# Attention on f32 operands as loaded, with first-layer tiles of 256 and four times 512 tokens, in a fused attention and two-MLP kernel

## What is computed

```
# attention: q, k, v are (4, 8, 576, 64), window 64
scores = scale * q @ k.T ; mask = (rel >= 0) & (rel < 64), else -1e9
attn   = softmax(scores) ; x = (attn @ v), heads side by side: (2304, 512)
# first MLP, d_ff 768
h = max(x @ w1, x @ w2, x @ w3) ; y = h @ w_out        # (2304, 512)
# second MLP, d_ff 2048
h = y @ w_in ; g = h if h >= 1, 0 if h <= -1, else (h + 1)**2 / 4
out = g @ w_out2                                       # (2304, 512)
```

## Time and profile before

| | |
|---|---|
| median of 3 runs | 801.43 us (801.33 to 801.45) |
| the profiled execution | 801.27 us, span of its records 799.1 us |
| PE busy | 772.5 us (97%), weight loads 705.2 us (88%) |
| DVE, ACT, POOL busy | 413.1 (52%), 407.2 (51%), 443.3 us (55%) |
| chain that ended last | PE 92%, DVE 3%, ACT 2% |
| transfers | 46.56 MB, 58 GB/s over the span |

### The profile page before, as it was taken

The page is one execution under the profiler, slowest core; times in us unless marked ns, Lnnn a source line. Parts: engine busy times, 40 slices in busy tenths (PEclk is TensorE's granted clock), DMA queues, the critical chain, the costliest instruction groups (busy, mean ns, idle before and its releaser), DMA issues.

```text
span 799.1 us, 12583 instructions
## 1 busy us (share of the span) xinstructions
PE 772.5 (97%) x4320; PEld 705.2 (88%) x4320; DVE 413.1 (52%) x903; ACT 407.2 (51%) x957; POOL 443.3 (55%) x371
## 2 busy tenths in 40 slices
PE   4689999999999999999999999999999999999997
PEld 4589999988888888899998988899998899998896
DVE  6677476644644521226316573374666456357434
ACT  7774778657566322043525455356555346345431
POOL 6867779755666326027517575266677457348221
PEclk9999999999999999999999999999999999999999
DMA  7621322321220021002001102002111001200302
GB/s 230 227 64 51 111 69 82 96 69 55 81 71 27 27 80 52 1 1 95 10 0 52 54 1 80 1 2 80 54 52 54 1 1 66 93 1 30 128 1 80
DMA packets 25193, 46.56 MB, mean 58 GB/s; under 512 B 2352, under 2 KB 5552, under 8 KB 25136
## 3 DMA queue, kind: packets, MB, share of 16 engines
q1 hardware_dynamic: 25136, 45.82, 17.2%
HBM read 37.95 MB, written 7.86 MB: 57 GB/s over the span
## 4 chain that ended last, share of the span: by engine, by line
PE 92%; DVE 3%; ACT 2%; DMA 1%; issue 1%; POOL 0%; SPq 0%; DVEq 0%; ACTq 0%
PE wide L563 28%; PE wide L635 24%; PE bank L615 22%; PE wide L588 8%; PE wide L547 3%; PE wide L526 3%; PE bank L538 2%; PE wide L549 1%; PE wide L528 1%; ACT prob L679 1%; DMA v_nat<-v_dram 1%; DVE prob L911 0%; DVE prob L904 0%; DMA raw<-w_dram 0%; DVE x_sums L929 0%
## 5 line engine op out<-in xcount | busy, mean ns | idle before, releaser
L563 PE MATMUL wide<-xT,w 128*128 128x256 f32 (+1 forms) x1296 | 240.8, 341 | 0.0
L563 PEld LDWEIGHTS wide<-xT,w 128*128 128x128 f32 x1296 | 199.8, 190 | 23.7
L635 PE MATMUL wide<-w4s,gT 128*128 128x512 f32 x864 | 210.1, 392 | 0.0
L1094 POOL TENSOR_TENSOR gT<-g,gT 128x384 fp32r<-128x384 f32 x96 | 105.5, 1109 | 178.4 <-ACT gT L652 178.4
L615 PE MATMUL bank<-yT,w3s 128*128 128x384 f32 x1008 | 188.1, 336 | 1.6 <-DVE g L1038 1.1
L635 PEld LDWEIGHTS wide<-w4s,gT 128*128 128x128 f32 x864 | 161.1, 188 | 31.2
L615 PEld LDWEIGHTS bank<-yT,w3s 128*128 128x128 f32 x1008 | 178.3, 188 | 7.7 <-DVE g L1038 1.5
L810 ACT ACTIVATE g_sq<-g_sq,half 128x384 f32<-128x384 f32 x96 | 58.1, 615 | 128.1 <-DVE g_sq L1033 127.7
L1021 DVE TENSOR_TENSOR pu<-bank,pu 128x384 f32<-128x384 f32 x72 | 40.1, 558 | 138.8 <-PE bank L615 131.0
L940 DVE TENSOR_TENSOR h<-wide,h 128x256 f32<-128x256 f32 (+1 forms) x72 | 40.1, 557 | 75.7 <-PE wide L563 75.3
L679 ACT ACTIVATE prob<-prob,neg_max 128x128 f32<-128x128 f32 x144 | 56.0, 390 | 41.4 <-DVE neg_max L911 41.2
(11 more groups left out here) (69 smaller groups left out, 972.5 us busy)
## 6 DMA issues: line engine op xcount, KB each, us to landing
v_nat<-v_dram SPq DMA_DIRECT2D x36, 256.0 KB, 2.6
raw<-w_dram SPq DMA_DIRECT2D x16, 512.0 KB, 3.5
h<-moe_w_dram SPq DMA_DIRECT2D x12, 384.0 KB, 6.6
out_dram<-o_sb SPq DMA_DIRECT2D x18, 256.0 KB, 2.1
k_in<-k_dram SPq DMA_DIRECT2D x12, 288.0 KB, 3.6
q_in<-q_dram SPq DMA_DIRECT2D x12, 256.0 KB, 2.9
part_dram<-o_sb SPq DMA_DIRECT2D x12, 256.0 KB, 2.1
part_in<-part_dram SPq DMA_DIRECT2D x2, 1536.0 KB, 7.3
```

The costliest lines, as they stand in the source:

```text
L563: mm = pe.matmul(acc[gr % 2][:, 0:cols], w123[:, wp, w, kc, c * P:(c + 1) * P], xT[:, x_side(t), xp, kc, 0:cols], start=(kc == x == 0), st ...
L635: mm = pe.matmul(acc4[b], gT[:, k, gp, tb * P:(tb + 1) * P], w4s[pair_f(g) % HALF_F][:, wp, f, :], start=(first and x == 0), stop=(last an ...
L1094: return pool.tensor_tensor(dst, src, high.bitcast(F32), ALU.subtract)
```

## The change

Attention's splits go: q, k and v are loaded straight into f32 buffers (four of each, `BUFS`) and PE multiplies them as f32, one matmul of 128 columns per block. Scores and values then have one half, so `mask`, `cross` and `x_sum` go too; the maximum reads PSUM and the mask itself, and both PSUM areas are double buffered. q is loaded by two transfers, one per head, each in pieces of 64 floats. `x_hi` and `x_lo` become two operations of 64 rows each, x_lo on DVE. Layer 1 has one tile of 256 and four of 512, and all order lists and due times are replanned. Besides: in the first period of layers 3 and 4, one copy of ACT comes earlier and one weight split goes to the next period; in the last unit DVE writes over `part_in` instead of `o_sb`, and the last block goes in two halves.

```diff
-PIECES = (1, 1, 1, 2, 2, 2)
+PIECES = (1, 2, 2, 2, 2)
+BUFS = 4
...
 FIRST = {
     "SP": """
-        k0 q0 mask0 v0 k1 q1 v1 k2 q2 k3 q3 v2 v3 w0 w1 w2 w3 k4 q4 w4 w5 w6 k5 q5 w7 v4 mask1 w8 k6 q6 w9
-        w10 w11 v5 k7 q7 v6 k8 q8 v7 k9 q9 v8
+        k0 q0 mask0 k1 q1 v0 k2 q2 v1 k3 q3 v2 v3 k4 q4 w0 w1 w2 w3 k5 q5 mask1 k6 q6 w4 w5 w6 v4 w7 k7 q7
+        v5 v6 w8 w9 v7 w10 w11 v8 v9 v10
     """,
     "PE": """
-        score0 score1 score2 probs0 values0 score3 probs1 probs2 values1 values2 probs3 values3 score4
-        score5 score6 group0 probs4 group1 group2 values4 group3 score7 group4 probs5 group5 group6
-        values5 group7 group8 probs6 group9 group10
+        score0 score1 score2 probs0 score3 probs1 values0 probs2 values1 values2 probs3 values3 score4
+        score5 group0 score6 group1 group2 probs4 score7 group3 probs5 score8 group4 values4 group5 probs6
+        score9 group6 values5 probs7 score10 group7 values6 group8 probs8
     """,
     "ACT": """
-        k_hi0 q_hi0 v_hi0 k_hi1 q_hi1 v_hi1 k_hi2 q_hi2 exp0 safe0 k_hi3 q_hi3 exp1 safe1 p_hi0 w_hi0 exp2
...
+        exp0 safe0 exp1 safe1 p0 exp2 safe2 p1 exp3 x_hi0 safe3 p2 x_hi1 w_hi3 x_hi2 p3 x_hi3 exp4 group0
+        safe4 exp5 group1 safe5 w_hi7 group2 p4 exp6 group3 safe6 p5 exp7 group4 safe7 w_hi9 x_hi4 group5
...
     "DVE": """
...
+        zeros0 zeros1 zeros2 zeros3 max0 max1 invert0 invert1 max2 invert2 max3 w_lo0 x_lo0 invert3 x_lo1
+        w_lo3 x_lo2 x_lo3 max4 w_lo4 max5 invert4 invert5 max6 max7 invert6 invert7 w_lo9 max8 x_lo4
...
     "POOL": """
...
+        norm0 norm1 norm2 w_hi0 w_hi1 w_hi2 norm3 w_lo1 w_lo2 w_hi4 w_hi6 norm4 w_lo6 norm5 w_hi5 w_lo5
...
         def q_in_of(n):
...
-            if n >= 2:
-                sp.wait_ge(*q_lo_by(n - 2))
-            sp.dma_start(q_in[:, n % 2, 0:cols], q_dram[:, u, start:start + cols]).then_inc(q_landed[n % 2], 16)
+            if n >= BUFS:
+                sp.wait_ge(scored, steps_of(n - BUFS)[1])
+            for h in range(2):
+                rows, _ = diagonal(h)
+                sp.dma_start(q2[rows, n % BUFS, 0:cols // BLK, h, :],
+                             q_dram[rows, u, start:start + cols].rearrange("p (j n) -> p j n", n=BLK)).then_inc(q_in[n % BUFS], 16)
...
         def score(s):
...
-            after(pe, mask_added, NB * (scores_before(s) + 1))
+            after(pe, maxed, NB * (s - 1))
             for b in range(NB):
...
-                pe.matmul(s_ps[:, b, :, :].rearrange("p x n -> p (x n)"), qT[:, n % 2, 0, j, :, :].rearrange("p h n -> p (h n)"),
-                          kT[:, n % 2, :, keys], start=True, stop=False, skip_group_check=True)
-                mm = pe.matmul(s_ps[:, b, 0, :], qT[:, n % 2, 1, j, :, :].rearrange("p h n -> p (h n)"),
-                               kT[:, n % 2, 0, keys], start=False, stop=True, skip_group_check=True)
+                mm = pe.matmul(scores_in[s % 2][:, b, :], q2[:, n % BUFS, j, :, :].rearrange("p h n -> p (h n)"),
+                               k2[:, n % BUFS, j * BLK:j * BLK + SPAN], start=True, stop=True, skip_group_check=True)
...
         def values(s):
+            pe.wait_ge(v_in[s % BUFS], 16 * (s // BUFS + 1))
+            pe.wait_ge(p_copied, s + 1)
+            after(pe, x_lo, 2 * (s - 1))
             for b in range(NB):
...
+                mm = pe.matmul(o_ps[s % 2][:, b, :], v2[:, s % BUFS, b, :], pT[:, s % 2, b * P:(b + 1) * P],
+                               start=True, stop=True, skip_group_check=True)
...
+        def x_hi_of(s):
             act.wait_ge(valued, s + 1)
...
+            for h in range(2):
+                rows, cols = diagonal(h)
+                hi(x_of(s, 0)[rows, :].rearrange("p (b n) -> p b n", b=NB), o_ps[s % 2][rows, :, cols]).then_inc(x_hi, 1)
...
+            if g_at == 1:
+                w3_parts(W3_IN[0], 2)
...
             if g_at == 0:
                 copy(g_at, 1)
                 square(g_at, 0)
+                copy(g_at, 2)
...
         def maxima(s):
...
             for b in range(NB):
-                dve.tensor_tensor_reduce(prob[:, s % 2, b, :], scores_of(s)[:, b, 0, :], prob[:, s % 2, b, :],
-                                         -SCALE, BIG, ALU.add, ALU.min, neg_max[:, s % 2, b:b + 1])\
-                    .then_inc(mask_added, 1)
+                dve.tensor_tensor_reduce(prob[:, s % 2, b, :], scores_in[s % 2][:, b, :], masks_of(s)[:, b, :],
+                                         -SCALE, BIG, ALU.add, ALU.min, neg_max[:, s % 2, b:b + 1]).then_inc(maxed, 1)
...
-            dve.tensor_tensor(o_sb[:, b % QB, :], acc4[b], part_in[:, b, :], ALU.add).then_inc(dve_out, 1)
+            cols = DM // 2 if unit == len(UNIT_PAIR) - 1 and b == BLOCKS - 1 else DM
+            for at in range(0, DM, cols):
+                dve.tensor_tensor(part_in[:, b, at:at + cols], acc4[b][:, at:at + cols], part_in[:, b, at:at + cols], ALU.add)\
+                    .then_inc(dve_out, 1)
```

## The result

The changed kernel takes 782.17 us (median of 6 runs, 778.73 to 783.81) against 801.44 beside it: ratio 0.975, 95% interval 0.9726 to 0.9773. That is faster, and 0.8 us from the 783 forecast. The profiled execution took 782.23 us, its span is 780.4.

What follows compares the result with a forecast made beforehand. PE bounds from 44.35 us on, vector work before. Start -17.0, score6 +0.9, f32 +2.5, tiles -2.8, gaps -0.8, first period -0.5, end -0.9 sum to -18.6 from 801.27: 783 us with the median; range 773 to 812.

Steps and rivals of the forecast that it cites:

- What bounds it: From 44.35 us on PE's work is the time; ahead of it vector work bounds, and only there its removal pays.
- The start: Ahead of layer 1's first group: without splits, scores begin earlier and group0 starts at 27.4 against 44.35 us, 17.0 less.
- its weakest number: In the start: about 4.6 MB ahead of weight w3 would take 22 us at 206 GB/s.
- The f32 block: Behind group0: 248 blocks at 0.24 us against 0.23, +2.5 us; bounds 0.09 and 0.46 us a block.
- score6: One step's scores fewer lie ahead of group0, so they fall behind it: +0.9 us.
- The tiles: Layer 1: two tiles of 256 become one of 512, matmuls 53.1 to 50.3 us: -2.8.
- The first period of layers 3 and 4: The copy comes earlier and the gap of 0.53 goes: -0.5 us; the moved split has a whole period before its product.
- The end: DVE's 0.84 us wait for a store out of `o_sb` goes and the last half block's store is shorter: -0.9.
- reloaded weights: Rival: each f32 pass loads its weights anew, a block costs about 0.46 us, 855 us in all; 13 in 100.
- loads hidden only in part: Rival: f32 blocks cost 0.30 to 0.38 us; 798 us at 0.30, 811 at 0.34; 12 in 100.
- a block at the transposes' price: Rival: an f32 block costs 0.12 us, nearly as cheap as a transpose, 753 us in all; 4 in 100.
- the start gives half: Rival: late weights, norm3 behind w_hi2 or q's small pieces put group0 at 36, 791 us in all; 12 in 100.

Runs made afterwards that it cites:

- the seven starts: Seven profiled executions with the same words up to group0: the changed kernel and six variants edited only behind the start; group0 begins at 26.00 to 30.43 us.
- the three prices above: Changed kernel with 96 extra f32 blocks of 128, 256 or 512 columns: 801.85, 821.11 and 863.21 us; a block costs 0.230, 0.432 and 0.858 us.

## Why the prediction was right

The sum was right to 0.1 us, but not by its terms: the start gave 2.1 us less than the text had, the f32 blocks 5.3 more, and several smaller misses, 3 us in all, made up the rest. That it came out so close was luck, also since the same kernel takes 779.1 us on average where it keeps its clock and 782.8 where it loses it for a while; the text had no term for that.

- **What bounds it**: right. Off DVE, ACT and POOL fell 66, 59 and 133 us of busy time; 14.9 of the 18.7 us are ahead of group0 and none of the rest comes of the vector engines but the 0.8 of gaps, which went as forecast. The text counted the first tile as covered; that holds with the vector work that is left, and not with 0.6 to 1.0 us a step more.
- **The start**: the mechanism was right as far as the runs separate it (the second PSUM area, which the text doesn't price, took waits of 4.8 us away too). The size was 2.1 us too large in this execution; in the seven starts group0 lies between 26.0 and 30.4, and the 27.4 of the text between them. Two things in "the start, worked through" failed. q's issues were taken at 0.45 us and are 0.60 to 0.72, and q1 landed at 8.43, so that score1 began at 8.52 (6.3 in the text). Only part of this is the issues: with the same ones q1 landed at 6.9 to 8.1 us in the other six starts. And norm0 was put at the end of exp0, but invert0 stands behind max1 on DVE: norm0 began at 11.71, probs0 at 12.89, not 10. The text named norm3 behind w_hi2 as what could be late, and it was: w0 to w2 landed at 18.5, 19.5 and 20.5, norm3 ended at 22.9 where the text put it at 19 to 20, and w3 landed at 21.8, as by the 22 us that the text called its weakest number. Against this the clock rose at 15.4 us and not with group0, which gave part of it back until it fell again.
- **The f32 block**: the choice between 0.09 and 0.46 us, four passes in two loads, was right. Only the size was off: 0.211 us on average in place of 0.24 (0.230 where one is added), and the old block averages 0.222 and not 0.23. This is from PE's starts between group0 and layer 2: 244 blocks take 54.1 us before, 248 take 52.2 after. With score6 the text had +3.4 for what measured -1.9. Of all terms this one was mis-sized most, by 5.3 us.
- **The tiles**: -2.8 in the text. The groups take 231.8 us before and 228.3 after, so -3.5, but 0.9 of this is the low clock of the first group before, a term that the text didn't have, and 0.8 the gaps. That leaves -1.7 between the two kernels; the run with the old tiles gives 3.1. The transposes take 0.4 more after than before.
- **The first period of layers 3 and 4**: wrong in sign, +1.0 for -0.5. The step "the moved split of chunk 2 has a whole period before its product" looked at the split's own consumer only. And the copy that comes earlier gained 0.1 and not 0.5: the gap of 0.53 ahead of layer 3 is gone, and one of 0.41 for POOL's gT stands ahead of layer 4. The chain of the kernel after shows the other:

```profile
412.45 2.95 POOL w3s L1003 x2
415.41 3.82 DMA raw<-w_dram
...
419.25 0.42 DVE s_sums L885
...
420.53 1.17 issue
421.70 0.56 DVE pu L928
...
422.30 1.32 PE bank L577 x6
```

  The split frees `raw3`, the next transfer waits for that, DVE's sums wait for the transfer, and DVE's add that PE needs stands behind them.
- **Layer 2**: +0.85 wasn't in the text. It comes of a transfer that takes 0.3 us longer and of a split on DVE that then began while POOL was at work, and not of the tiles.
- **The end**: -0.7 for -0.9.

The rivals: reloaded weights, loads hidden only in part and a block at the transposes' price are out by the three prices above. Of "the start gives half" the mechanism was there, at 2 us and not at 8. That q's 256 B pieces slow the transfers is seen in the packets: in the first 30 us one of 256 B took 22 ns on average, one of 1,024 B in the kernel before 51, which is 1.7 times as long for a byte. The rule that the text names for it, of the Trainium skill (DMA: Bandwidth & Descriptors, Specifications), agrees with this. For the 0.8 MB of q ahead of w3 this is an estimated 1.7 us of all 16 engines. How much of it reaches group0 no run separates from the longer issues; the one that took four issues off SP got back what the issues alone explain.

## What to carry to other kernels

Where vector engines prepare operands for PE and PE is idle for it only at the start, count the start and not the busy shares; and price a full f32 matmul as four times its columns, which at 128 columns is no more than two matmuls on high and low parts (0.21 against 0.22 us a block here). With fixed orders a late transfer holds every word behind the one that waits for it: mending one engine moved the same wait to the next, twice, and with all of them mended the bound was the weights' own splits. Before a start is tuned, see how far it differs between executions of one kernel; here it was 4.4 us, more than any edit of the start gave. When a word that frees a buffer is moved later, follow the buffer to its next transfer and to what stands behind that transfer's first reader.

## What the runs showed of the hardware

- One f32 matmul appears as two weight loads and two matmul records. The distance of records is 111 to 112 ns at 128 columns, 216 at 256 and 429 at 512, at the full clock.
- PE's clock rose between 8.7 and 16.9 us in all 13 profiled starts of the changed kernel and its variants, and fell again to half in nine of them, for 3.4 to 13.7 us, with gaps of PE beside or ahead of it; the same kernel kept it in some executions and lost it in others (778.73 and 783.81 us). In layers 3 and 4 a gap of 1.2 us in one execution and gaps of 0.9 and 0.8 in another were followed by a fall of 3.4 us that cost 1.6, where like gaps in others were not.
- A transfer issue on SP took 0.43 us for k (128 rows of one piece) and 0.60 to 0.72 for half of a q of 256 tokens (64 rows of four pieces). The issue right behind a q took longer as well: 0.60 for a v behind it, 0.43 for a v behind a v.
- An operation of DVE that began while POOL was at work took longer. The low part of one weight (128x768) took 0.95 to 0.96 us in each of the 23 cases in 13 traces in which POOL was idle when it began, and 0.96 to 2.57 in the others; the low part of h1 took 2.55 us without and 3.08 with POOL at work.
